# Unit 1's scores in two dense banks, its last pair first and its keys transposed before the mix

## What is computed

```python
for t in range(S):                                   # recurrence, per batch and head
    cur = einsum('bhd,bhe->bhde', u[None] * kt, vt)
    y[:, :, t] = einsum('bhd,bhde->bhe', rt, state + cur)
    state = wt[..., None] * state + einsum('bhd,bhe->bhde', kt, vt)
# first layer, x is y with the heads side by side
xk = mu_k * x + (1 - mu_k) * x_prev;  xr = mu_r * x + (1 - mu_r) * x_prev
k = maximum(xk @ w_k, 0);  x = sigmoid(xr @ w_r) * (k * k @ w_v)
# second layer: gelu(x @ w_in) in halves u, v; v normalised, mixed over time by w_sg
out = x + (u * v_s) @ w_out
```

## Time and profile before

| | |
|---|---|
| median of 3 runs (lowest to highest) | 333.68 us (333.19 to 333.71) |
| the profiled execution, its own time | 332.61 us |
| its span | 330.9 us |
| PE busy | 320.0 us, 97% of the span, 2684 matmuls |
| PEld, loads of the standing operand | 299.5 us, 91% |
| DVE busy | 197.2 us, 60% |
| ACT busy | 151.0 us, 46% |
| POOL busy | 98.1 us, 30% |
| PE in the chain that ended last | 84% |

### The profile page before, as it was taken

The page is one execution under the profiler, slowest core; times in us unless marked ns, Lnnn a source line. Parts: engine busy times, 40 slices in busy tenths (PEclk is TensorE's granted clock), DMA queues, the critical chain, the costliest instruction groups (busy, mean ns, idle before and its releaser), DMA issues.

```text
span 330.9 us, 6786 instructions
## 1 busy us (share of the span) xinstructions
PE 320.0 (97%) x2684; PEld 299.5 (91%) x2684; DVE 197.2 (60%) x331; ACT 151.0 (46%) x301; POOL 98.1 (30%) x94
## 2 busy tenths in 40 slices
PE   6987899999999999999999999999999999999996
PEld 2657889999999999999999998899999988999996
DVE  4869999983696398639416055991643546123432
ACT  5446844553845455465547592755113025311100
POOL 5530344004314211430032050672233018313220
PEclk9999999999999999999999999999999999999999
DMA  7979033232304401300006036000000210000012
GB/s 230 408 259 350 27 124 125 87 130 61 144 2 165 166 5 24 144 9 2 6 9 240 0 110 246 29 0 0 2 0 0 97 49 0 2 0 2 0 48 95
DMA packets 11153, 28.09 MB, mean 85 GB/s; under 512 B 1232, under 2 KB 5872, under 8 KB 9840
## 3 DMA queue, kind: packets, MB, share of 16 engines
q1 hardware_dynamic: 10976, 27.51, 23.7%
q10 hardware_dynamic: 144, 0.14, 0.1%
HBM read 24.74 MB, written 2.36 MB: 82 GB/s over the span
## 4 chain that ended last, share of the span: by engine, by line
PE 84%; DVE 7%; ACT 3%; issue 2%; DMA 2%; POOL 0%; SPq 0%; ACTq 0%; DVEq 0%
PE pm L297 16%; PE pm L298 15%; PE pm L299 15%; PE ps L613 3%; PE ps L297 3%; PE ps L299 3%; PE ps L298 3%; PE py L691 3%; PE pkt L638 3%; PE py L677 2%; PE pkt L297 2%; PE pkt L299 2%; PE pu L297 2%; PE pu L299 2%; PE pkt L298 2%
## 5 line engine op out<-in xcount | busy, mean ns | idle before, releaser
L542 POOL TENSOR_TENSOR k_l<-sq,k_h 128x512 fp32r<-128x512 f32 x24 | 31.9, 1332 | 79.2 <-ACT sq L944 79.2
L297 PE MATMUL pm<-xkr_h,wk_h 128*128 128x256 f32 x144 | 42.1, 292 | 0.0
L297 PE MATMUL pm<-k_h,wv_h 128*128 128x256 f32 x144 | 41.2, 286 | 0.4 <-POOL k_l L542 0.4
L299 PE MATMUL pm<-k_h,wv_l 128*128 128x256 f32 x144 | 40.7, 283 | 0.0
L298 PE MATMUL pm<-k_l,wv_h 128*128 128x256 f32 x144 | 40.7, 283 | 0.0
L298 PE MATMUL pm<-xkr_l,wk_h 128*128 128x256 f32 x144 | 40.7, 283 | 0.0
L299 PE MATMUL pm<-xkr_h,wk_l 128*128 128x256 f32 x144 | 40.7, 282 | 0.0
L533 POOL TENSOR_TENSOR rkp<-inw 128x512 f32<-128x512 f32 x12 | 15.3, 1281 | 62.7 <-DVE r_in L1132 62.7
L936 ACT ACTIVATE relu<-pm 128x512 f32<-128x512 f32 x24 | 14.3, 596 | 36.2 <-PE pm L299 36.1
L595 POOL TENSOR_TENSOR gated_l<-gf,gated_h 128x384 fp32r<-128x384 f32 x16 | 16.4, 1025 | 46.1 <-ACT gated_h L1055 36.1
L1187 DVE SCALAR_TENSOR_TENSOR xf<-X,omu,xf 128x256 f32<-128x256 f32 x36 | 19.5, 554 | 15.4 <-ACT xf L902 15.4
(11 more groups left out here) (239 smaller groups left out, 880.4 us busy)
## 6 DMA issues: line engine op xcount, KB each, us to landing
inw<-in_units SPq DMA_DIRECT2D x10, 1026.5 KB, 5.0
vb<-in_vT SPq DMA_DIRECT2D x12, 256.0 KB, 5.0
wsg_raw<-in_wsgT SPq DMA_DIRECT2D x1, 2304.0 KB, 8.8
out_y<-y_out SPq DMA_DIRECT2D x12, 192.0 KB, 1.9
wk_raw<-in_moe_w_k SPq DMA_DIRECT2D x3, 512.0 KB, 9.9
wv_raw<-in_moe_w_v SPq DMA_DIRECT2D x4, 384.0 KB, 7.0
win_raw<-in_moe_w_in SPq DMA_DIRECT2D x3, 512.0 KB, 4.6
inw<-in_units SPq DMA_DIRECT2D x2, 512.0 KB, 5.5
```

The source lines that it names most:

```text
L297: pe.matmul(o, a_h, b_h, start=first and n == 0, stop=False, skip_group_check=True)
L299: mm = pe.matmul(o, a_l, b_h, start=False, stop=last and n == len(pairs) - 1, skip_group_check=True)
L542: pool.tensor_tensor(k2_l[:, 2 * n:2 * n + 2], sq[:, j % 2].rearrange("p (g t) -> p g t", g=2), k2_h[:, 2 * n:2 * n + 2], ALU.subtract).th ...
```

## The change

- The scores of unit 1 go to banks 0 and 1 of a new PSUM tensor `dense`, whose three banks are what `pm` was; they no longer wait for unit 0's mask. All other scores stay in `ps`.
- The bonus of unit 0 goes to `pkt`, that of unit 1 to the second bank of `ps`.
- The last pair of unit 1's output goes to the first bank of `ps`. PE makes it ahead of the other three pairs and tells DVE by a semaphore of its own, `last_mm`; DVE's `last_output(1)` waits for that alone.
- `keys_by_step(1)` follows `move_last(1)` directly, and one of the three warm-up products behind it is gone.
- ACT's `keys(1)` stands inside the mix of stage 0.
- Scores of unit 2 and later wait for the outputs and bonuses of units 0 and 1 too.

```diff
-            return pm[un] if un < 2 else pkt
+            return ps[:, 1] if un == 1 else pkt[:]
+        def score_banks(un):
+            return dense[:, 0:2] if un == 1 else ps[:]
+        def last_bank(un):
+            return ps[:, 0, 0:C] if un == MOVED else y_bank(un)[:, MAIN:WIDE]
...
                 pe.wait_ge(rin_done, un + 1)
-                if un:
+                if un >= 2:
                     pe.wait_ge(att_done, un)
+                    pe.wait_ge(bonus_done, 2)
+                    pe.wait_ge(y_done, 2)
...
-                if un > 2:
+                if un:
                     pe.wait_ge(bonus_done, un)
...
                 pe.wait_ge(rkp_done, un + 1)
-                if un >= 2:
+                if un == 1:
+                    pe.wait_ge(att_done, 1)
+                else:
                     pe.wait_ge(ktok_done, states(un + 1))
                     pe.wait_ge(bonus_done, un)
...
             from_chunk(0)
-            from_state(1)
             bonus(1)
-            from_chunk(1)
+            for pairs, done in ((range(PAIRS - 1, PAIRS), last_mm), (range(PAIRS - 1), y_mm)):
+                from_state(1, pairs)
+                from_chunk(1, pairs, done)
             move_last(1)
+            keys_by_step(1)
             pe.wait_ge(y_done, 1)
             pe.wait_ge(main_done, 1)
-            warm(pe, 3)
+            warm(pe, 2)
...
                     for tile in RS:
                         first_mlp(s, *tile)
-                    keys_by_step(1)
                     add_state(1)
...
                 for i in range(1, len(MIXES)):
                     part_now(s, *MIXES[i])
                     mix_high(s, *MIXES[i - 1])
+                    if s == 0 and i == KT:
+                        keys(1)
...
                     gate(s, *RS[1])
-                    keys(1)
                     high_weight(wv[1])
...
                 values = inw[:, un % 3, VF]
-                dve.wait_ge(y_mm, un + 1)
                 dve.wait_ge(bonus_done, un + 1)
                 if un == MOVED:
+                    dve.wait_ge(last_mm, 1)
                     last_output(un)
                     low_part(dve, parts_of("wk")[1], wl2_done)
                     dve.wait_ge(moved_mm, 1)
+                dve.wait_ge(y_mm, un + 1)
```

More of the change, by code:

```diff
@@ L208, in build @@
             "prod_done", "inv_done", "suffix_done", "rkp_done", "rin_done", "kin_done"))
[L209 to L210 removed]
+        c_mm, kt_mm, sc_mm, u_mm, y_mm, flag_mm, last_mm, moved_mm = (sem(n) for n in (
+            "c_mm", "kt_mm", "sc_mm", "u_mm", "y_mm", "flag_mm", "last_mm", "moved_mm"))
         bonus_done, ktok_done, att_done, main_done, y_done = (sem(n) for n in (
@@ L292, in warm @@
             for _ in range(times):
-                pe.matmul(pm[2][:], ident[:], one[:, 0:512], start=True, stop=True)
+                pe.matmul(pm[2], ident[:], one[:, 0:512], start=True, stop=True)
         def three(pe, o, pairs, first, last):
@@ L612, in scores @@
                         head = slice(h * SLOT, (h + 1) * SLOT)
-                        mm = pe.matmul(ps[:, h, cols], k_in[head, p, cols], r_in[head, p, cols], start=True, stop=True)
+                        mm = pe.matmul(score_banks(un)[:, h, cols], k_in[head, p, cols], r_in[head, p, cols], start=True, stop=True)
                 mm.then_inc(sc_mm, 1)
@@ L663, in add_state, with y_place, from_state @@
                 mm.then_inc(u_mm, 1)
-            def from_state(un):
+            def y_place(un, g):
+                return last_bank(un) if g == PAIRS - 1 else y_bank(un)[:, g * C:(g + 1) * C]
+            def from_state(un, pairs=range(PAIRS)):
                 if place(un)[2] == 0:
@@ L672, in from_state @@
                     pe.wait_ge(main_done, un)
-                for g in range(PAIRS):
+                for g in pairs:
                     cols = slice(g * C, (g + 1) * C)
@@ L676, in from_state, with from_chunk @@
                         head = slice(h * SLOT, (h + 1) * SLOT)
-                        pe.matmul(y_bank(un)[head, cols], state[head, (un - 1) % 2, g], r_in[head, un % 2, cols],
-                                  start=g == 0, stop=False, skip_group_check=True)
-            def from_chunk(un):
+                        pe.matmul(y_place(un, g)[head], state[head, (un - 1) % 2, g], r_in[head, un % 2, cols],
+                                  start=g == pairs[0], stop=False, skip_group_check=True)
+            def from_chunk(un, pairs=range(PAIRS), done=y_mm):
                 first = place(un)[2] == 0
@@ L687, in from_chunk @@
                     pe.wait_ge(main_done, un)
-                for g in range(PAIRS):
+                for g in pairs:
                     cols = slice(g * C, (g + 1) * C)
                     for h in range(2):
-                        mm = pe.matmul(y_bank(un)[h * SLOT:(h + 1) * SLOT, cols], vb[:, un % 3, g, h, :],
-                                       att[:, un % 2, h, cols], start=first and g == 0, stop=g == PAIRS - 1,
+                        mm = pe.matmul(y_place(un, g)[h * SLOT:(h + 1) * SLOT], vb[:, un % 3, g, h, :],
+                                       att[:, un % 2, h, cols], start=first and g == pairs[0], stop=g == pairs[-1],
                                        skip_group_check=True)
-                mm.then_inc(y_mm, 1)
+                mm.then_inc(done, 1)
             def move_last(un):
```

17 lines of the change are left out of this document (9 added, 8 removed).

## The result

| | before | after |
|---|---|---|
| median of 7 runs (lowest to highest) | 333.68 us (333.04 to 333.84) | 332.15 us (331.79 to 332.88) |
| ratio, 95% interval | | 0.9967 (0.9955 to 0.9979) |
| the profiled execution, its own time | 332.61 us | 332.15 us |
| its span | 330.9 us | 330.4 us |
| PE busy | 320.0 us, x2684 | 320.4 us, x2682 |

By the medians the change makes the kernel 1.5 us faster (0.46%). By the ratio, which isn't that of the two medians, it is 0.33%, 1.1 us (0.7 to 1.5). The forecast was 0.1 us. Between the two profiled executions there are only 0.5 us. The rest is in executions of the kernel before that its first profile doesn't show. This is the key to the case, and experiment e1 opens it.

What follows compares the result with a forecast made beforehand. It took DVE's unbroken chain to unit 2's mask, started by a transfer's landing, to set when PE's unbroken stretch begins near 41 us. Only the landing gained, 0.1 us, the rest 0: 333.68 - 0.1, about 333.6 us, range 332.6 to 334.3.

Steps and rivals of the forecast that it cites:

- rivals 1 and 4: Rival 1: the 2.1 us hole was on the path, 331.1 us, 7%. Rival 4: keys copy delays mix, 334.3 us, 5%.
- What the profile stood for: Profiled execution, 332.61 us, lay 1.07 us below the runs' median; the gain of 0.1 was taken from the median, 333.68.
- The hole of 2.1 us, gain 0: PE's wait for copied keys: moves to two later places, gain 0 at 41.2 us, bounds 0 and 2.1.
- Rival 3: PE's clock falls in its pauses; 1.7 us lost if in the last one, 335.3 us; 8%.
- The mix starts with the landing, 0.1: Unit 0's last pair landing in X starts the mix; it lands 0.1 us earlier, bounds 0 and 0.2.
- Rival 2: Start of the mix: unit 1's X is last, not the transfer; gain 0.4 to 0.7 us, 333.1 us; 18%.
- The lag has a cause that every run has: Argument against rival 2: the lagging DMA engine, read from a 16 KB instruction packet costing it 1.0 us.
- Unit 1's X, 21.5: Unit 1's X ends near 21.5 us, 0.5 earlier, by moving its last pair first; covered by the landing.
- DVE's wait of 0.9 for ACT: DVE's one wait of size from 22 to 42 us, for ACT's first multiplication of the mix.
- Copy inside the mix, warm-up product: ACT's key copy, 0.59 us, hidden by its waits, cost 0; removing a 0.9 us warm-up product doesn't move DVE.
- Behind 41.2: PE's nearly unbroken stretch after 41.2 us: same instructions, same order; only the moment it begins changes the total.
- Its own signs: Unit 2's mask within 0.3 us of 41.07, X near 21.5; wrong if mask before 40.5 or clock below 1.0 behind 24.

Runs made afterwards that it cites:

- e1: The kernel before, run again with no edit: 333.36 us, ratio 0.9994; the clock fell in 10 of 12 runs.
- e4: The kernel before with two warm-up products put into PE's wait of 2.1 us for the copied keys: 332.65 us, no fall in 12 runs.
- e3: The kernel before with only the transposes of unit 1 and ACT's key copy moved early: 332.55 us, ratio 0.9976.
- e9: The changed kernel, run again with no edit: 332.03 us, ratio 0.9972 to before; the clock fell in 8 of 12 runs.
- e2: The changed kernel with unit 1's transposes and ACT's key copy put back behind the gate tiles: 332.63 us, ratio 0.9976 to before.
- e5: The kernel before with only the change's banks, bonuses and their waits, plus DVE's second wait before unit 1's X: 333.03 us, ratio 0.9995.
- e6: The kernel before with one redundant wait in DVE's queue in front of unit 1's X: 332.77 us, ratio 0.9993.
- e7: The changed kernel with DVE's low part of the first quarter of w_v moved behind the mask of unit 2: 331.62 us.
- e13: The kernel before with the keys moved early and one redundant DVE wait before unit 1's X: 332.17 us, ratio 0.9971.
- e14: The changed kernel without DVE's second wait for the sums in front of unit 1's X: 332.64 us, ratio 0.9984 to before.
- e10: The changed kernel with the third warm-up product ahead of the first stage put back: 331.90 us, ratio 0.9970 to before.
- e8: The changed kernel with DVE's w_v low part behind unit 2's mask and two warm-up products before unit 2's scores: 331.17 us, no fall.
- e11: The changed kernel with two warm-up products in PE's wait before the scores of unit 2, DVE's order unchanged: 331.94 us, no fall.
- e12: The kernel of e8 with one of the four warm-up products at the very start removed: 331.18 us, no fall.

## Why the prediction was wrong

It said 333.6 us, within 332.6 to 334.3; it is 332.15. (The times of rivals 1 and 4 start from 333.68 instead of 333.6, a slip of 0.1 us that decides nothing.) By its steps:

**What the profile stood for.** "That one was 1.07 us below the median of the runs" was put into the sum as an offset and not asked about. It was the finding. The executions that make the median have a fall of PE's clock that the profiled one has not. This is the step that failed first, and the next one hangs on it. Filling the pause, with all work left in its place, takes the falls away and 0.7 us off the median (e4).

**The hole of 2.1 us, gain 0.** In the execution shown this holds to a tenth: PE's hole moved to the scores, the mask of unit 2 set the start of the stretch, and moving the keys gained nothing there. In e3 and e9, whose clock held, PE has 1.3 and 1.4 us in hand ahead of the mask (I had 1.2). But in 75 of 110 runs of before the clock falls. In the execution of before with a fall that was traced (e1) PE comes 0.83 us behind the mask instead of 0.15, and so it is, by 0.83 to 0.91 us, in the other three traces with the keys late and a fall (e2, e5, e6); what the moved keys give PE is then on the path. Rival 3 had the mechanism and the price, half of 3.4 us less the slack, and it said that a fall at 31 us is mostly hidden with the change. I tied it to the pauses that the change adds, counted one pause before where the earlier trace rows has 0.8 and 0.6 us beside it, and took one pause without a fall as a sign that it doesn't fall. It falls before and after the change alike. The change pays for it. The term that I set to 0 measured 0.8 us (e3), and 0.7 from the other side (e4).

**The mix starts with the landing, 0.1.** The landing is at 22.12 us in the trace of after and at 22.13 before, though issued 0.1 us earlier. There the rule of the Trainium skill (DMA: Bandwidth & Descriptors, Queues, rings and completion order) gave the right number. It can be chance, since the last landing lies anywhere from 21.05 to 22.31 us in the 16 traces. It is at 21.89 in e1 and at 21.56 us in e9, with unit 1's X last, at 22.34 and 22.37. X releases the mix in 12 of the 16 traces, the transfer only in before, after, e6 and e7. Rival 2, at 18%, is what happens in most. "The lag has a cause that every run has" was wrong: the packet of instructions that I blamed stands in all 16 traces between 18 and 20 us and takes about 1.0 us of one DMA engine in each, but the second transfer took 3.5 to 3.6 us only in before, after and e7, and 2.2 to 3.2 us in the others. What makes it late stays open.

**Unit 1's X, 21.5.** It ends at 21.01 + 0.56 = 21.57 us. DVE's low part took 2.00 us instead of 1.22 because it began inside POOL's, which ended at 19.81 us; it ended 1.1 us after that. The Trainium skill (SBUF — State Buffer, Who interferes with whom) says that a VectorE instruction with both inputs in SBUF contends with a GpSimd one that reads SBUF, and the row agrees. But that isn't what set X. The low part was over at 20.91 us, PE's products that move the last pair only at 20.04 + 0.94 = 20.98, and X began at 21.01. In e9 the low part took 1.34 us, and DVE stood 0.77 us for those products. I had them start near 19.8; so 21.5 came out right for another reason than mine. Counted from the scores of unit 0, X ends after 13.07 us here and 13.08 in e9, and after 13.52 and 13.30 in the two traces of before: 0.2 to 0.45 us gained, not 0.5. On the total it is the smallest term, about 0.1 (e13 against e9).

**DVE's wait of 0.9 for ACT.** I read it as one wait. About 0.4 of it was a gap between the release and the start, and one wait more in the queue takes it away (e6), one less brings it back (e14). No step of the prediction had this.

**Copy inside the mix, warm-up product.** Both cost 0, as forecast (DVE's mix runs at its old pace from 22.84 on; e10).

**The sum put right**, against medians: 0.7 to 0.8 for the keys, 0.4 for the wait, 0.1 to 0.3 for X, together 1.2 to 1.5 us. Measured 1.53 and, in e9's group, 0.98 us; by the ratios 1.1 and 0.9. So the sum may be some tenths too high. In e9's group the kernel before had fewer falls, 16 of 29, and its two kinds of runs have medians 0.9 us apart.

**Behind 41.2.** In all 16 traces, of before, after and e1 to e14, the time from the first product with unit 2's masked scores to the end of the span is 289.6 to 289.7 us. That part of the reading, that only this moment counts, held throughout.

**Its own signs.** The mask of unit 2 ended at 40.62 us, outside the 0.3 around 41.07 but not before 40.5. The granted clock fell to 0.50 behind 24 us, which I had named as a sign of being wrong. X at 21.57 and ACT's start by the transfer, at 22.22, came as forecast in this execution.

## What to carry to other kernels

If the profiled execution is faster than the median by more than the runs scatter, look for what the others have: the granted clock of each run, beside its time, showed it at once. A wait that isn't on the path in one trace can be what makes the clock fall, or what is missing to absorb a fall, in the next; price slack on TensorE with a fall in it. Filling a wait with idle products is a cheap test of this, and here it was worth as much as moving the work.

## What I had not expected of the hardware

- The clock fell in 75 of 110 runs of the kernel before and in none of the 36 of the four kernels with a filled wait (e4, e8, e11, e12). The Trainium skill (TensorE: Matmul & The Clock Gate, Part 1) says that the clock falls back when the engine is idle, and the runs agree in that the falls vanish with the pause. One pause of 2.1 us led to a fall in some executions and to none in others. In the eight traces with a fall it began between 0.1 us before and 0.9 us behind the end of that pause.
- In the traces the clock first rose between 5.7 and 8.5 us. The late rises put the scores of unit 0 at up to 9.3 us instead of 8.4. With the keys early, the four traces with an early rise have the fall and the three with a late one have none.
- One redundant wait in DVE's queue moved an instruction by 0.4 us, by a mechanism that is still open.
